# Attention and two gated products, one core: the probabilities of the last three pairs of heads beside batch 0 turned in 32x32 blocks and moved by DMAs

## What is computed

```
scores = cap * tanh(q @ k.T / sqrt(64) / cap)
attn   = exp(scores - max(scores)) / (sum(...) + 1e-9)
x      = attn @ v                               # all heads beside each other: 768 columns
x      = (sigmoid(x @ w_gate) * (x @ w_val)) @ w_out      # 768 -> 1536 -> 768
h      = x @ w_in                                          # 768 -> 2048
y      = (h * cos(h)) @ w_out2                             # 2048 -> 768
```

## Time and profile before

| | |
|---|---|
| median of 3 runs | 1212.66 us |
| the profiled execution | 1212.74 us |
| its span (first to last instruction) | 1210.7 us |
| TensorE's mean granted clock | 0.999 of full speed |
| busy: PE, VectorE, ScalarE, GpSimd | 99%, 52%, 42%, 43% |
| DMA | 298.8 MB, mean 247 GB/s |

### The profile page before, as it was taken

The page is one execution under the profiler, slowest core; times in us unless marked ns, Lnnn a source line. Parts: engine busy times, 40 slices in busy tenths (PEclk is TensorE's granted clock), DMA queues, the critical chain, the costliest instruction groups (busy, mean ns, idle before and its releaser), DMA issues.

```text
span 1210.7 us, 16764 instructions
## 1 busy us (share of the span) xinstructions
PE 1198.8 (99%) x5932; PEld 1089.7 (90%) x5932; DVE 628.4 (52%) x1227; ACT 508.5 (42%) x957; POOL 516.0 (43%) x458
## 2 busy tenths in 40 slices
PE   7999999999999999999999999999999999999998
PEld 6779999999899999999999999989999999999998
DVE  8951158866773467876651265777662211105610
ACT  8941155655641355555640245545661011105610
POOL 7969968789653346661103405664302100000000
PEclk9999999999999999999999999999999999999999
DMA  4579986799776698989678769999769666666663
GB/s 158 163 242 323 321 303 234 242 335 322 264 286 236 226 266 258 260 256 287 236 232 281 246 200 259 270 272 258 259 228 279 194 222 218 211 220 221 239 232 110
DMA packets 150034, 298.77 MB, mean 247 GB/s; under 512 B 60480, under 2 KB 69440, under 8 KB 149952
## 3 DMA queue, kind: packets, MB, share of 16 engines
q1 hardware_dynamic: 134064, 287.37, 72.3%
q10 hardware_dynamic: 15888, 10.33, 3.2%
HBM read 219.39 MB, written 58.98 MB: 230 GB/s over the span
## 4 chain that ended last, share of the span: by engine, by line
PE 94%; DVE 2%; ACT 1%; SPq 1%; DMA 1%; issue 0%; ACTq 0%
PE acc L824 27%; PE acc L823 26%; PE acc L825 26%; PE s_ps L721 3%; PE s_ps L722 2%; PE acc L776 2%; PE t_ps L793 2%; PE t_ps L795 1%; PE t_ps L758 1%; PE t_ps L742 1%; PE acc L813 1%; SPq L466 1%; PE acc L815 1%; DVE rowmax L1424 1%; DMA pt_lo_whole<-h_lo_whole 0%
## 5 line engine op out<-in xcount | busy, mean ns | idle before, releaser
L823 PE MATMUL acc<-h_hi,w_hi 128*128 128x448 f32 x672 | 247.4, 368 | 0.0
L824 PE MATMUL acc<-h_lo,w_hi 128*128 128x448 f32 x672 | 245.7, 366 | 0.0
L825 PE MATMUL acc<-h_hi,w_lo 128*128 128x448 f32 x672 | 245.5, 365 | 0.0
L823 PE MATMUL acc<-x_hi,w_hi 128*128 128x448 f32 x576 | 211.0, 366 | 0.0
L824 PE MATMUL acc<-x_lo,w_hi 128*128 128x448 f32 x576 | 210.6, 366 | 0.0
L825 PE MATMUL acc<-x_hi,w_lo 128*128 128x448 f32 x576 | 210.6, 366 | 0.0
L544 POOL TENSOR_TENSOR pt_lo<-pt_lo_whole,pt_hi 128x1344 fp32r<-128x1344 f32 x24 | 74.5, 3102 | 224.7 <-ACT pt_hi L1046 224.7
L823 PE MATMUL acc<-z_hi,w_hi 128*128 128x448 f32 x384 | 140.4, 366 | 0.0
L825 PE MATMUL acc<-z_hi,w_lo 128*128 128x448 f32 x384 | 140.2, 365 | 0.0
L824 PE MATMUL acc<-z_lo,w_hi 128*128 128x448 f32 x384 | 140.2, 365 | 0.0
L825 PEld LDWEIGHTS acc<-h_hi,w_lo 128*128 128x128 f32 x672 | 126.2, 188 | 10.2
(11 more groups left out here) (138 smaller groups left out, 1984.1 us busy)
## 6 DMA issues: line engine op xcount, KB each, us to landing
w_lo<-w_pair SPq DMA_DIRECT2D x156, 384.0 KB, 4.0
w_hi<-w_pair SPq DMA_DIRECT2D x156, 384.0 KB, 3.5
w_lo_whole<-w SPq DMA_DIRECT2D x52, 384.0 KB, 4.0
w_pair<-w_lo SPq DMA_DIRECT2D x52, 384.0 KB, 4.5
w_pair<-w_hi SPq DMA_DIRECT2D x52, 384.0 KB, 5.0
w_lo<-w_pair SPq DMA_DIRECT2D x36, 512.0 KB, 4.5
w_hi<-w_pair SPq DMA_DIRECT2D x36, 512.0 KB, 3.8
qk_in_whole<-qk SPq DMA_DIRECT2D x35, 512.0 KB, 5.7
```

The lines of the kernel that those rows point to most:

```text
L823: e.matmul(out[:, 0:S], w_hi[u % HI][:, wb, :], a_hi[:, kb, :], start=first, stop=False)
L824: e.matmul(out[:, 0:S], w_hi[u % HI][:, wb, :], a_lo[:, kb, :], start=False, stop=False)
L825: return e.matmul(out[:, 0:S], w_lo[u % LO][:, wb, :], a_hi[:, kb, :], start=False, stop=last)
```

## The change

`MOVED` becomes 9: the last three pairs beside batch 0 (pairs 9, 10, 11; i = 3, 4, 5) go the second way. Their low parts are made by VectorE (a new `moved_low` there), their DMAs are issued by SP (`moves_of_first`) and ScalarE (a general `move_blocks`). i = 3 is turned before the third product, moved and made into high and low parts within it; i = 4 and 5 pass through `turned_z` in the fourth product. From step 12 on scores run five groups ahead instead of four (`AHEAD_4`); group 16's scores come between the second and third product. `split_qk` and `load_qk` of i = 4 come earlier.

```diff
-MOVED = 2 * PAIRS
+MOVED = PAIRS + PAIRS // 2
+FOURTH_0 = 2 * U2
+AHEAD_4 = AHEAD + 1
...
-    def ahead(b):
-        return MOVED_AHEAD if b > 0 else AHEAD
+    def ahead(b, n):
+        return MOVED_AHEAD if b > 0 else AHEAD if n < FOURTH_0 else AHEAD_4
+    def beside_h(b):
+        return BESIDE_H if b > 0 else FOURTH_0 // NG + 1
+    def turned_by_tensor(b, n):
+        return 0 <= n < STEPS and group_of(b, n) < NG * MOVED
+    def turned_at(b, n):
+        g = n + ahead(b, n) - 2
+        if b == 0 and (g < FOURTH_0 or n == FOURTH_0):
+            return None
+        return g if 0 <= g < STEPS else None
+    def high_beside_third(b):
+        return (1, 2) if b > 0 else (3, 5)
... SP
-                if stage == 3 and h == 0 and j in (0, 2):
+                if stage == 2 and n == 11:
                     for d in range(2):
-                        load_qk(first + 4 + j // 2, d)
+                        load_qk(first + 4, d)
+                if stage == 3 and h == 0 and j == 2:
+                    for d in range(2):
+                        load_qk(first + 5, d)
+            def moves_of_first(n):
+                first = halves.index((3, 1, 1))
+                if 0 <= n - first < 4:
+                    move_blocks(pair_of(0, FOURTH_0 // NG), (n - first) // 2, ((n - first) % 2,))
+                i, r = divmod(n - halves.index((4, 2, 1)), NG)
+                i += FOURTH_0 // NG + 1
+                if n >= halves.index((4, 2, 1)):
+                    if r in (0, 2):
+                        move_blocks(pair_of(0, i), r // 2, (0, 1, 2) if n == len(halves) - 1 else (0, 1))
+                    else:
+                        move_blocks(pair_of(0, i), r // 2, (2,))
                             keep(*halves[n - KEEP_LATER])
+                        moves_of_first(n)
... GpSimd
-                if stage == 3 and h == 1 and j in (0, 2):
-                    split_qk(first + 4, j // 2)
+                if stage == 3 and j == 0:
+                    split_qk(first + 4, h)
... TensorE, attend
-                if b == 0 and n == 2 * U2:
-                    e.wait_ge(s_r2, b * KF2 + KF2 - 2)
-                if b == 0 and 0 <= n + 1 < STEPS:
+                if turned_by_tensor(b, n + 1):
                     transposes(group_of(b, n + 1))
                 blocks(1)
                 if i >= 0 and r in (1, 3):
-                    if b == 0:
+                    if pair_of(b, i) < MOVED:
                         times_v(b, i, r // 2)
                     else:
                         times_v_moved(b, i, r // 2)
... TensorE, after long_product(b, 2)
+                if b == 0:
+                    between = group_of(b, FOURTH_0 + AHEAD)
+                    e.wait_ge(s_tanh, between)
+                    scores(between, s_ps)
... ScalarE, attend
-                if b > 0 and n % 2 == 0 and 0 <= n + 2 < STEPS and n != FOURTH:
+                if n % 2 == 0 and 0 <= n + 2 < STEPS and (n != FOURTH if b > 0 else n > FOURTH_0):
                     move_last_blocks(b, n)
-                if b == 0 and 0 <= n + 1 < STEPS:
+                if turned_by_tensor(b, n + 1):
                     pt_high(group_of(b, n + 1))
...
-                i, r = divmod(n + 1, NG)
-                if b > 0 and 0 <= i < PAIRS and r in (0, 2) and i != FOURTH // NG:
+                i, r = divmod(n + 1 if b > 0 else n, NG)
+                if 0 <= i < PAIRS and r in (0, 2) and pair_of(b, i) >= MOVED and i != first_of_fourth(b) // NG:
                     moved_high(pair_of(b, i), r // 2)
... ScalarE, second_product (the Exp and Tanh stand around z_high) and third_product
+                if b == 0:
+                    exp(group_of(b, FOURTH_0 + AHEAD - 1))
+                if b == 0:
+                    tanh(group_of(b, FOURTH_0 + AHEAD))
+                    if b == 0 and j < 4:
+                        move_blocks(pair_of(b, FOURTH_0 // NG), j // 2, 2 + j % 2)
+                    if heads_beside(b) and j in high_beside_third(b):
+                        moved_high(pair_of(b, first_of_fourth(b) // NG), high_beside_third(b).index(j))
... VectorE
+            def moved_low(pr, d):
+                e.wait_ge(s_pbhi, 2 * (pr - MOVED) + d + 1)
+                at = of_head(d)
+                e.tensor_tensor(pt_lo[:, 0:CH, at], pt_whole[:, 0:CH, at], f32(pt_hi)[:, 0:CH, at],
+                                ALU.subtract).then_inc(s_pblow, 1)
+                e.wait_ge(s_pblow, 2 * (pr - MOVED) + d + 1)
+                e.tensor_tensor(pt_hi[0:D, CH, at], pt_whole[D:P, CH, at], f32(pt_hi)[D:P, CH, at],
+                                ALU.subtract).then_inc(s_pb, 1)
             def attend(b, n):
+                g = turned_at(b, n)
+                if b == 0 and g is not None:
+                    turn_blocks(group_of(b, g))
+                i, r = divmod(n, NG)
+                if b == 0 and FOURTH_0 // NG < i < PAIRS and r in (1, 3):
+                    moved_low(pair_of(b, i), r // 2)
... VectorE, end of second_product, and third_product
+                if b == 0:
+                    last = FOURTH_0 + AHEAD - 1
+                    normalise(group_of(b, last), zeros[0])
+                    for g in (last - 1, last):
+                        turn_blocks(group_of(b, g))
+                    row_max(group_of(b, last + 1))
+                    if b == 0 and j in high_beside_third(b):
+                        moved_low(pair_of(b, FOURTH_0 // NG), high_beside_third(b).index(j))
```

More of the change, by code:

```diff
@@ L862, in attend @@
                 i, r = divmod(n, NG)
[L863 to L864 removed]
+                if n + ahead(b, n) < STEPS:
+                    g = group_of(b, n + ahead(b, n))
                     e.wait_ge(s_tanh, g)
```

55 lines of the change are left out of this document (26 added, 29 removed).

## The result

| | before | after |
|---|---|---|
| median of 4 runs each | 1212.55 us (1211.05 to 1213.18) | 1230.18 us (1226.35 to 1231.37) |
| ratio of the runs | 1 | 1.0142, 95% interval 1.0117 to 1.0167 |
| profiled execution, its span | 1212.74, 1210.7 us | 1231.37, 1229.5 us |
| TensorE's mean granted clock | 0.999 | 0.992 |

The kernel became 17.6 us slower, where 5 us less were forecast. The 75 transposes are gone: the page, part 1, against the earlier trace rows.

A forecast was written before the change was run, and what follows sets the result against it. TensorE, busy 99% of the span, was taken as the bound. From 1212.74 us, -8.25 for transposes, -0.4 at the fourth product's start and +3.6 for low-part waits gave 1207.7 us, range 1204.0 to 1212.5.

The forecast's parts named there:

- What leaves TensorE: Three pairs beside batch 0 lose 75 transposes on TensorE at 0.110 us each: -8.25 us.
- The start of the fourth product: Before step 13's scores TensorE waits 1.31 us for a Tanh, but earlier holes of 0.95 and 0.74 go: -0.4 us.
- The durations of the low part: VectorE's two subtractions per moved head take 1.6 us (large) and 0.6 us (small), 2.2 us together.
- The waits behind them: TensorE waits for low parts in steps 17, 19 and 21 for 1.4, 1.3 and 0.9 us: +3.6 us.
- port: GpSimd's subtractions hold up VectorE's three late low parts, up to 2.4 us each: 1207.7 plus 0 to 7.2 us; chance 0.19.
- What the queues take over: 96 small DMAs on SP and ScalarE, and half 40's load 7.6 us late, were costed at nothing.
- The room behind the DMA share: DMA engines, 0.92 busy at 325 GB/s in the third product, could carry more, as another window shows 420.
- the low price: In the third product a move costs 0.14 us by its bytes; 32 moves take 4.5 us.
- Starved: SP and the DMA engines fall behind in the third product: 1212.6 us at low price, 1228 at high; chance 0.14.
- both prices: Kernel times if third-product queues fall behind: 1212.6 us with 32 moves at 4.5 us, 1228 us at 20 us.
- Clean: Fourth-product waits of 3.6 us fall away: 1204.1 us, or 1204 to 1206 with batch 1's first weights late; chance 0.22.

The follow-up runs named there:

- e14: Changed kernel with third and fourth products reordered, four of SP's moves per head on ScalarE, batch 1's loads awaiting only their own buffer's stores; 1211.8 us.
- e5: Changed kernel with pair 3's moves spread, two per half on SP without the wait, two per unit on ScalarE, last parts in unit 6; 1228.0 us.
- e3: Changed kernel with 12, 6 and 12 filler matmuls on TensorE ahead of the late products of steps 17, 19 and 21; 1230.5 us.
- e4: Changed kernel with GpSimd writing zeros by a one-input operation in place of its subtraction in the fourth product; 1232.0 us.
- e9: As e5, but the high and low parts of pair 3's head 1 come in steps 13 and 14, out of the third product; 1221.1 us.
- e1: Changed kernel with SP's moves of pair 3 two halves later, at half 41's place instead of half 39's; 1232.3 us.
- e6: As e5, but SP's moves begin at half 39's place again, so SP waits for turned blocks ahead of half 40's load; 1225.1 us.
- e2: Changed kernel with pair 3's 32 moves carrying one element each, same places and number of issues; 1228.8 us.
- e13: Changed kernel with third and fourth products reordered, and four of SP's twelve fourth-product moves per head issued by ScalarE; 1215.6 us.

## Why the prediction was wrong, by its own steps

Waits are from start to start here, as the prediction counts them.

- **What leaves TensorE: right.** 75 instructions less. That they are worth what was counted shows only once most waits are gone: e14's fourth product is 2.6 us shorter than before with 4.4 us of waits and 2.8 of slow clock in it.
- **The start of the fourth product: right in kind.** A wait of 1.77 us ahead of step 13's scores, 1.31 forecast. It grows to 5.9 us when a high and a low part are put into unit 6 (e5).
- **The durations of the low part: right** (1.54 and 0.62 us undisturbed, 1.6 and 0.6 forecast). **The waits behind them: too small**: 3.15, 1.90 and 3.27 us against 1.4, 1.3 and 0.9. The rival "port" came true on top of the forecast (4.2 us for step 17's two subtractions), and in step 20 ScalarE's four issues took 4.0 us where I had 2.8 from rows of a calmer stretch. The Trainium skill (SBUF — State Buffer, "SBUF: two separate sides") had it as a rule that a VectorE operation with two SBUF inputs and a GpSimd operation that reads SBUF keep each other out, and the trace agrees: 2.65 for 0.62 us, and GpSimd's own 3.72 for 2.41. It should have been a term of the sum and not a rival.
- **The clock: no step of the prediction had it.** At the waits of steps 17 and 21, 3.0 and 3.1 us idle, the granted clock fell, and 5.6 us were lost by it. The waits of 1.4 and 1.7 us idle in the same kernel lost none; that of 2.2 us in the third product lost 1.5. e3 shows that it hangs on TensorE's idleness; what else decides it is open, as the 1.85 us of e4 and the 2.90 us of e9 show.
- **What the queues take over: this step failed**, where it says "I cost all this at nothing". Its facts were right (SP's wait until 244, 245.7 measured; half 40's load at 247, 248.5 measured), its price was not: 8.6 us in the third product. The error that a run shows alone stands in its last but one sentence, that ScalarE's issues "fill the 3 us that it is idle in each unit". Three issues had taken 2.18 us; four took 4.0 to 4.2 in three of four units, and the idle time lay between a unit's halves, not ahead of both. In e1 it is what TensorE waits for: units of 9.4 us. On SP the same: four issues between two loads, 2.7 to 3.9 us, in a half of 3.65. e5 against e1 prices the bursts on both queues, with unit 5's parts, at 5.4 us, and e6 against e5 prices SP's wait at some 1.5.
- **The room behind the DMA share: not there.** The share went to 0.99 at 349 GB/s and not to 420. ScalarE's queue, which carries 16 moves and nothing else from 246 to 304 us (queue: packets, MB, share of the engines' time):

```profile
q1 hardware_dynamic: 8124, 17.59, 87.3%
q10 hardware_dynamic: 2048, 0.80, 5.6%
```

  5.6% of 58 us is 3.2 us, 0.20 us per move by its bytes where 0.14 was the low price: 246 GB/s, against 348 for the other queue. The Trainium skill (DMA: Bandwidth & Descriptors, "Specifications") says that transfers under 512 bytes miss the line rate; these rows have 448, and the lower rate fits it. The two queues differ in more than the length of their rows (these blocks go from SBUF to SBUF, the weights to and from DRAM), so no run shows how much of it is due to the length. And e2 shows that in the third product the bytes were not the cause.
- **The rivals** were made as cases that exclude each other. Starved and port came together, and 1230 lies outside the range and above both prices. Clean named the first weights of batch 1 as the next bound at up to 2 us: not seen in the changed kernel, which came too late for it, and up to 5.7 us in most kernels that came sooner.

What stays open: the 2.8 us of the changed kernel behind the start of batch 1 (three waits of 0.7 to 0.9 us for a Tanh and one of 0.4 us for weights stand in its trace, against one of 0.6 before; not followed further), what besides TensorE's idleness decides when the clock falls, how the 5.4 us of the bursts divide between the two queues, and why executions choose 93.07 or 94.57 us for the first product.

## What to carry to other kernels

Work taken from an engine that is 99% busy is worth its time only if each queue that takes over has slack at that very place in its order: look for the idle time between two given instructions, not for an engine's or a DMA share's sum. A DMA issue is an instruction of its engine, and its length must be taken from transfers of the same size in a stretch with the same DMA load. Where several queues are near full in one stretch, removing one cause shows nothing or moves the wait to the next; take them away together before you call one innocent.

## What the runs showed of the hardware that was not expected

- A move's issue took 0.6 to 0.7 us on ScalarE in a calm stretch, 1.0 us in the mean of three groups of four where the DMA share was 0.92 to 1.03, and 2.0 us in e13 (two in 4.0 us, DMA share 1.02). One-element moves took 0.6 to 0.8 us each at a share just as high (0.72 to 1.03), so the length needs both, the load and the bytes. A fourth group of full moves took only 2.9 us at a share of 0.98, so a group can escape it.
- GpSimd holds VectorE up with a one-input operation too: in e4 VectorE's large subtraction, 1.54 us, took 2.32 beside it, and GpSimd's copy of v, 0.4 us, took 1.7.
- The clock can be held at its upper level through a wait: with 12 matmuls ahead of it, into a bank that is overwritten anyway, the granted clock stayed at 1.00 in e3. Step 17 still waited 0.7 us behind them, so they delayed nothing there.
- The clock can fall at a wait shorter than one that leaves it alone: 1.85 us (e4, clock 0.79 over 8 us) against 2.90 us (e9, 1.00).
